# Attention and routing in one kernel: score bursts that begin one double earlier, with the split double first, and everything that hangs on their order

## The chip, the cores and the metric

One core of one Trainium2 chip runs the whole kernel. The metric is the device time of one execution in microseconds; the span is the time from the first to the last instruction of the profiled one.

## What is computed

```
# u, v: (8, 3072, 256), z: (8, 3072, 64)
scores = matmul(z, z.transpose(0, 2, 1)) / 3072
attn = maximum(scores, 0) ** 2
x = (u * matmul(attn, v)).reshape(24576, 256)
# then: 8 experts, first come first served, 768 rows each
logits = x @ w_gate;  expert = argmax(logits);  gate = softmax(logits)[expert]
row i goes to its expert if fewer than 768 rows came before it
out[i] = gate[i] * (maximum(row @ w1[expert], 0) @ w2[expert]), else 0
```

## The kernel before

The attention is made in groups of 384 rows (three tiles of 128), eight groups to a batch. A group has 12 **doubles**: a double is two chunks of 128 keys. For each double TensorE makes scores (two of 128 keys by 384 rows), ScalarE a relu and a square (`do_relu`, `do_square`), VectorE a float16 high half and a low half (`do_hi`, `do_lo`), and TensorE then weighs the values with them: for each of the three tiles six matmuls of 256 columns (`weigh`), which add up in two banks of PSUM, `O`. There are four buffers for a double (`BUFS`).

Scores are made in bursts of four doubles, in the six other banks, `Sc`. Three of the four doubles take two banks each, 384 columns wide; the fourth lies in thirds of 128 columns behind them (`score_place`). A burst stands ahead of double 0, 4 and 8 of a group, and makes the scores of the doubles four further on: the one ahead of double 8 makes doubles 0 to 3 of the next group, with queries and keys that GpSimd has copied aside (`q_next`, `k_next`), since the batch may change there. The rest of a group's scores use `q_now`. A burst may begin when the relus of the burst before are done.

The rows of a finished group are routed while the next group is computed, on the same engines. In order: `gate_x` (VectorE scales the outputs by u, L1074 and L1078), three sums of absolute values (ScalarE, L543), the row scale (VectorE, L1112 to L1118), high halves of the rows (ScalarE, L553), low halves (VectorE, L1128), three transposing DMAs (SyncE, L292), the gate logits (TensorE, L817, behind double 3), VectorE's choice of an expert (L1173 to L1183), the counts (TensorE, L759 and L762, behind the burst ahead of double 4), the slots, and three scattering DMAs of GpSimd (L426). A flag says whether all experts are full; the engines read it behind double 4 (`load_end`), and this data fills them in group 18. The second part of the program, the experts' matrices (from L848 on), then begins.

During groups 4 to 7 and 12 to 15 (`g > 3`) the next batch is split into halves: values (`v_high`, `v_low`) and keys (`keys_high`, `keys_low`). Keys are needed on both halves of the partitions, so each half is also made or copied across. In groups 3 and 11 the scales for it come from `norms`, four matmuls whose sums lie in a bank of the scores. Groups 4 to 11 also scale and split the first experts' weights.

`wait_apart` waits on a semaphore and counts once in another; `only_if` is a branch. "c" in the functions is the double at which an engine's program stands, "n" the group, K0 = 12 n. Each engine runs its own list in order, and no scheduler moves anything.

```
behind = n * 11 + (c - 3 if c > 3 else c - 2)      # do_hi waits for TensorE's use of the buffer
act.wait_ge(s["scores_ready"], K + 1)              # do_relu
wait_apart(act, s["lo_done"], K - BUFS + 1)
```

## Time and profile before

| what | value |
|---|---|
| median of three runs | 865.88 us (865.76 to 866.64) |
| profiled execution | 866.84 us, its span 865.0 us |
| mean granted clock of TensorE in it | 0.993 of 2.4 GHz |
| relu of a double, ScalarE | 803 ns |
| square of a double, ScalarE | 837 ns |
| high half, low half of a double, VectorE | 556 ns, 959 ns |
| output matmul of 256 columns | 273 ns long, 109 ns from start to start |
| a fetch of queries, issue to landing | 2.1 us |

An engine's operations overlap by some 0.1 us at their ends, so the distance from start to start is what counts. Group n's first output matmul follows group n - 1's last with one burst between. The attention takes about the first 608 us, the experts the rest.

### The profile page before, as it was taken

The page shows a single profiled execution, that of the slowest core. Times are in us where ns is not written, and L with a number is a line of the kernel's source. Part 1 is how long each engine was busy: PE and PEld are TensorE (multiplying, and loading weights), DVE is VectorE, ACT ScalarE, POOL GpSimd, SP SyncE. Part 2 cuts the span into 40 slices and gives each one's busy share as a digit, 9 for nine tenths or more (in the row PEclk, how much of TensorE's full clock was granted, in tenths as well). Part 3 has the DMA queues.
Part 4 walks back from the last instruction along what each step waited for, and adds up shares of the span by engine and source line. Part 5 has one row for each costly group of instructions (what it writes and reads, how often), then busy time and mean ns, then how long its engine had stood idle before and what let it go on. Part 6 is the DMA issues. An engine that isn't in the chain of part 4 may idle for free.

```text
span 865.0 us, 25707 instructions
## 1 busy us (share of the span) xinstructions
PE 838.2 (97%) x8358; PEld 667.9 (77%) x8358; DVE 631.4 (73%) x1359; ACT 562.3 (65%) x873; POOL 171.3 (20%) x204
## 2 busy tenths in 40 slices
PE   6799999999999999999999999999999999999997
PEld 5688887888888788787888888888677777777776
DVE  7777877898888888987888888687464655565521
ACT  7867796687778779776778778577334434435422
POOL 3002113112212202202202411220122121211212
PEclk8999999999999999999999999999999999999999
DMA  8923236136243733323323413832625325415201
GB/s 293 338 84 110 75 121 225 49 120 219 64 130 110 245 120 109 117 65 109 114 68 118 146 50 117 313 75 51 128 80 171 96 87 158 142 46 152 55 18 36
DMA packets 108119, 106.53 MB, mean 123 GB/s; under 512 B 68493, under 2 KB 94298, under 8 KB 107072
## 3 DMA queue, kind: packets, MB, share of 16 engines
q1 hardware_dynamic: 99360, 85.71, 32.1%
q0 software_dynamic: 8736, 20.51, 6.8%
q8 instruction: 14, 0.23, 0.1%
q14 instruction: 9, 0.07, 0.0%
HBM read 40.03 MB, written 44.93 MB: 98 GB/s over the span
## 4 chain that ended last, share of the span: by engine, by line
PE 80%; issue 6%; DVE 6%; DMA 2%; SPq 2%; ACT 1%; DVEq 1%; ACTq 0%; POOL 0%; POOLq 0%
PE Sc L868 14%; PE O L747 13%; PE O L749 13%; PE O L751 13%; PE Sc L708 12%; PE O L891 3%; PE O L895 3%; PE O L893 3%; DVE attn_hi L1027 2%; PE Sc L895 2%; PE Sc L893 2%; PE Sc L891 2%; SPq L292 1%; DMA xT<-xrow 1%; PE O L817 1%
## 5 line engine op out<-in xcount | busy, mean ns | idle before, releaser
L747 PE MATMUL O<-vS,attn_hi 128*128 128x256 f16 x1326 | 362.0, 273 | 0.2 <-issue 0.2
L749 PE MATMUL O<-vS,attn_hi 128*128 128x256 f16 x1326 | 361.5, 273 | 0.0
L751 PE MATMUL O<-vS,attn_lo 128*128 128x256 f16 x1326 | 361.4, 273 | 0.0
L514 ACT ACTIVATE attn<-Sc 128x768 f32<-128x768 f32 x225 | 176.9, 803 | 113.1 <-PE Sc L708 71.7
L1033 DVE TENSOR_TENSOR attn_lo<-attn,attn_hi 128x768 f16<-128x768 f32 x222 | 212.8, 959 | 13.6 <-issue 6.6
L518 ACT ACTIVATE attn<-attn 128x768 f32<-128x768 f32 x225 | 184.5, 837 | 1.5
L747 PEld LDWEIGHTS O<-vS,attn_hi 128*128 128x128 f16 x1326 | 129.6, 98 | 30.9 <-issue 15.3
L426 POOL DMA_INDIRECT disp<-xrow,slot x54 | 66.4, 1230 | 390.3 <-DVE slot L1211 379.4
L751 PEld LDWEIGHTS O<-vS,attn_lo 128*128 128x128 f16 x1326 | 129.8, 98 | 15.1
L749 PEld LDWEIGHTS O<-vS,attn_hi 128*128 128x128 f16 x1326 | 129.8, 98 | 14.3
L1339 DVE SCALAR_TENSOR_TENSOR rawv<-Sc,rawv 128x768 f16<-128x768 f32 x63 | 60.1, 956 | 109.7 <-ACT rawv L629 71.3
L1027 DVE CAST attn_hi<-attn 128x768 f16<-128x768 f32 x223 | 123.9, 556 | 19.8 <-PE O L751 9.1
L629 ACT ACTIVATE rawv<-Sc 128x768 f16<-128x768 f32 x63 | 51.0, 810 | 100.9 <-PE Sc L868 97.0
L708 PE MATMUL Sc<-q_now,zP 64*128 64x128 f16 (+1 forms) x648 | 77.0, 269 | 4.8 <-issue 4.8
L868 PE MATMUL Sc<-vS,w1h 128*128 128x384 f16 x384 | 78.0, 326 | 0.3 <-DVE rawv L1339 0.3
L708 PE MATMUL Sc<-q_now,zQ 64*128 64x128 f16 (+1 forms) x648 | 76.4, 270 | 0.0
L891 PE MATMUL O<-w2s,rawv 128*128 128x256 f16 x256 | 69.8, 273 | 0.0
L895 PE MATMUL O<-w2s,rawv 128*128 128x256 f16 x256 | 69.8, 273 | 0.0
L893 PE MATMUL O<-w2s,rawv 128*128 128x256 f16 x256 | 69.8, 273 | 0.0
L466 POOL DMA_INDIRECT out<-attn,vS x48 | 47.1, 981 | 113.9 <-ACT attn L641 100.7
L708 PEld LDWEIGHTS Sc<-q_now,zP 64*128 64x128 f16 x648 | 46.0, 94 | 18.0 <-issue 9.8
L868 PEld LDWEIGHTS Sc<-vS,w1h 128*128 128x128 f16 x384 | 37.5, 98 | 21.5 <-issue 0.5
(167 smaller groups left out, 1070.1 us busy)
## 6 DMA issues: line engine op xcount, KB each, us to landing
out<-empty SPq DMA_DIRECT2D x16, 1536.0 KB, 5.9
wraw<-in_moe_w SPq DMA_DIRECT2D x16, 1024.0 KB
rawv<-in_v SPq DMA_DIRECT2D x14, 768.0 KB, 7.7
ubuf<-in_u SPq DMA_DIRECT2D x19, 384.0 KB, 3.2
disp<-vS SPq DMA_DIRECT2D x8, 774.0 KB, 10.5
rawz<-in_z SPq DMA_DIRECT2D x3, 768.0 KB
q_now<-zP POOLq DMA_DIRECT2D x18, 96.0 KB, 2.1
q_now<-zQ POOLq DMA_DIRECT2D x18, 96.0 KB, 1.9
```

The source lines that it names most:

```text
L514: act.activation(attn_place(c), score_place(c), ACT.Relu).then_inc(s["relu_done"], 1)
L518: act.activation(attn[:, c % BUFS, :, :], attn[:, c % BUFS, :, :], ACT.Square, scale=ROOT_C).then_inc(s["square_done"], 1)
L708: ins = nc.tensor.matmul(to, keys[r], queries[r][:, columns], start=at == 0, stop=at == len(terms) - 1)
L747: nc.tensor.matmul(o_part(t), hi, v[:, 0:D], start=c == 0 and j == 0 and t % 2 == 0, stop=False, skip_group_check=True)
L749: nc.tensor.matmul(o_part(t), hi, v[:, D:2 * D], start=False, stop=False, skip_group_check=True)
L751: ins = nc.tensor.matmul(o_part(t), lo, v[:, 0:D], start=False, stop=c == PAIRS - 1 and j == 1, skip_group_check=True)
L868: ins = nc.tensor.matmul(Sp[:, 2 * (p % 2) + fi, 0:GROUP], w[par][:, m, f * P:(f + 1) * P], xt[k][:, x + m, :], start=(at == 0), stop=(at ...
L891: nc.tensor.matmul(y_part(t), hi, w2s[:, par, f, 0:D], start=f == 0, stop=False, skip_group_check=True)
L893: nc.tensor.matmul(y_part(t), hi, w2s[:, par, f, D:2 * D], start=False, stop=False, skip_group_check=True)
L895: ins = nc.tensor.matmul(y_part(t), lo, w2s[:, par, f, 0:D], start=False, stop=f == FC - 1, skip_group_check=True)
L1027: dve.tensor_copy(attn_hi[:, b, :, :].rearrange("p j n -> p (j n)"), attn[:, b, :, :].rearrange("p j n -> p (j n)")).then_inc(s["hi_done"], 1)
L1033: dve.tensor_tensor(attn_lo[:, b, :, :], attn[:, b, :, :], attn_hi[:, b, :, :], ALU.subtract).then_inc(s["lo_done"], 1)
```

## The change

All of it moves work or waits; the arithmetic is the same.

- A burst begins one double earlier: ahead of double 0 it now makes doubles 3 to 6, ahead of 4 doubles 7 to 10, ahead of 8 doubles 11 and 0 to 2 of the next group. The double in thirds comes first. All four count as ready together, at the burst's end. Only three doubles are scored ahead of the first group, which need one slice of keys, not two, and 90 empty matmuls follow, not 50.
- VectorE makes the halves of double c + 3 at double c, not c + 2, and its extra work of a double stands ahead of them. Behind the scaling of the rows comes only the high half of double 2; its low half follows the row scale.
- ScalarE makes the rows' high halves ahead of the first relu, and relu and square stand one double later.
- The logits stand between the second and the third tile of double 3, whose tiles go in the order 2, 0, 1.
- The norms lie in the free columns of an output bank, as twelve matmuls of 128 columns behind double 7; TensorE waits for their use ahead of tile 2 of double 8.
- The copies of the new keys across, one on ScalarE and one on VectorE, become two DMAs of SyncE behind its flag wait. `khi_ready` and `klo_ready` count by 16.
- GpSimd fetches `q_now` behind the burst ahead of double 8, with `q_next`.
- VectorE makes the low half of double 6 at the end of the routing, ahead of the flag.

```diff
         def score_place(c):
-            i = c % BURST
-            if i < BURST - 1:
-                return Sp[:, 2 * i:2 * i + 2, 0:GROUP]
+            i = (c + 1) % BURST
+            if i:
+                return Sp[:, 2 * i - 2:2 * i, 0:GROUP]
...
+            def across(to, h, made_parts):
+                own, out = half(h), half(1 - h)
+                for hi_or_lo, made, copied in ((0, "zhi_ready", "khi_ready"), (1, "zlo_ready", "klo_ready")):
+                    own16, to16 = ((zP, zQ), (zQ, zP))[(h + hi_or_lo) % 2]
+                    wait_apart(sp, s[made], made_parts)
+                    sp.dma_start(to16[out, bass.ds(to, SLICE * P)], own16[own, bass.ds(to, SLICE * P)]
+                                 ).then_inc(s[copied], 16)
...
                 def rest():
-                    wait_apart(pool, s["scores_ready"], n * PAIRS + PAIRS)
-                    queries(q_now, n + 1, "loaded_q_now")
                     wait_apart(pool, s["scattered"], n * 48)
...
-                    wait_apart(pool, s["scores_ready"], n * PAIRS + PAIRS + BURST)
+                    wait_apart(pool, s["scores_ready"], n * PAIRS + PAIRS + BURST - 1)
+                    queries(q_now, n + 1, "loaded_q_now")
                     queries(q_next, n + 2, "loaded_q_next")
...
             def do_relu(K, c):
-                act.wait_ge(s["scores_ready"], K + 1)
+                act.wait_ge(s["scores_ready"], K - c + (c + 1) // BURST * BURST + BURST - 1)
...
-                        do_square(K0 + c + BURST, c + BURST)
+                        if c % BURST == 0:
+                            do_relu(K0 + c + 3, c + 3)
+                        do_square(K0 + c + 3, c + 3)
+                        if c % BURST != BURST - 1:
+                            do_relu(K0 + c + 4, c + 4)
...
-            wait_keys(4, False)
-            burst(0, 0, 0, 0)
-            turn_over(50)
+            wait_keys(2, False)
+            for c in range(BURST - 1):
+                ins = scores(0, c, 0)
+            ins.then_inc(s["scores_ready"], BURST - 1)
+            turn_over(90)
...
                         elif c == 0 and not peeled:
                             wait_apart(pe, s["loaded_q_now"], n * 32)
                             wait_keys((n & 120) + 6)
-                            wait_apart(pe, s["relu_done"], K0 + BURST)
-                            burst(K0 + BURST, n, BURST, par)
+                            wait_apart(pe, s["relu_done"], K0 + BURST - 1)
+                            burst(BURST - 1)
...
                                 wait_apart(pe, s["loaded_k_next"], ((n + 1) & 120) * 8 + 64)
-                                only_if(pe, g == 3, lambda: wait_apart(pe, s["nrm_done"], (n & 120) + 8))
...
-                        for t in range(TILES):
+                        for t in (TILES_LAST if c == LOGITS_AT[0] else range(TILES)):
...
+                            if not peeled and (c, t) == (2 * BURST, 2):
+                                only_if(pe, g == 3, lambda: wait_apart(pe, s["nrm_done"], (n & 120) + 8))
...
-                                    norms(zsq).then_inc(s["nrm_psum"], 8)
+                                    for k in range(PAIRS):
+                                        squares = nc.tensor.matmul(next_norm_sums, onesb[:, :], zsq[:, k * P:(k + 1) * P],
+                                                                   start=False, stop=k == PAIRS - 1, skip_group_check=True)
+                                    squares.then_inc(s["nrm_psum"], 8)
...
                         if c == PAIRS - 1:
                             gate_x(n + 1)
-                        if peeled or c != ROUTE_AT + 1:
-                            do_hi(K0 + c + 2, c + 2, n)
-                        do_lo(K0 + c + 2, c + 2)
+                            do_hi(K0 + c + 3, c + 3, n)
                         if not peeled and c == ROWS_LO_AT:
+                            do_lo(K0 + 2, 2)
...
+                        if not peeled and c == ROUTE_AT:
+                            route_rows()
+                        elif c < PAIRS - 1:
+                            do_hi(K0 + c + 3, c + 3, n)
+                            do_lo(K0 + c + 3, c + 3)
...
-FIRST_BURST_AT = 2
-RELUS = ((4,), (4, 5), (5,), ())
+FIRST_BURST_AT = 1
-LAST_KEYS_AT = 2
+LAST_KEYS_AT = 1
-NRM_AT = 7
+NRM_AT = 8
-ZHI_AT = (8, 9)
-ZLO_AT = 9
+ZHI_AT = 7
+ZLO_AT = 8
-LOGITS_AT = (3, 2)
+LOGITS_AT = (3, 0)
+TILES_LAST = (2, 0, 1)
```

On VectorE, from the row scale at the beginning of a group to the low halves of the rows, its program before reads (`rinv` and `rscale` are the row scale, `attn_hi` and `attn_lo` the halves of a double, `xrow` the rows):

```order
L1115 TENSOR_SCALAR rscale<-rinv 128x3
L1118 TENSOR_SCALAR rowfac<-rinv,ginv 128x3
L230 REGISTER_ALU
L1026 ISA
L1027 CAST attn_hi<-attn 128x768
L1033 TENSOR_TENSOR attn_lo<-attn,attn_hi 128x768
L1127 ISA
L1128 SCALAR_TENSOR_TENSOR xrow<-ubuf,rscale,xrow 128x256
```

and of the change:

```order
L1187 TENSOR_SCALAR rscale<-rinv 128x3
L1190 TENSOR_SCALAR rowfac<-rinv,ginv 128x3
L1057 ISA
L1058 TENSOR_TENSOR attn_lo<-attn,attn_hi 128x768
L1198 ISA
L1199 SCALAR_TENSOR_TENSOR xrow<-ubuf,rscale,xrow 128x256
```

The high half of that double has moved up, to directly behind the scaling of the outputs, and the double that stood there before has moved ahead of the scaling.

On ScalarE, from the sums at the beginning of a group, before:

```order
L543 ACTIVATE xrow,l<-ubuf 128x256 x3
L511 ISA
L230 REGISTER_ALU
L514 ACTIVATE attn<-Sc 128x768
L553 ACTIVATE xrow<-ubuf,rscale 128x256 x3
L518 ACTIVATE attn<-attn 128x768
```

and now, where the relu shown is that of the double in thirds:

```order
L559 ACTIVATE xrow,l<-ubuf 128x256 x3
L564 ACTIVATE xrow<-ubuf,rscale 128x256 x3
L530 ISA
L533 ACTIVATE attn<-Sc 128x3x2x128
L536 REGISTER_ALU
L537 ACTIVATE attn<-attn 128x768
```

The rows' high halves (`xrow` from `rscale`) stand ahead of the relu now.

On TensorE, around the logits (`wgs` are the gate's weights, `O<-vS` output matmuls, `Sc` scores), before:

```order
L749 MATMUL O<-vS,attn_hi 128x256
L751 MATMUL O<-vS,attn_lo 128x256
L230 REGISTER_ALU
L817 MATMUL O<-wgs,xT 128x16 x12
L230 REGISTER_ALU x2
L708 MATMUL Sc<-q_now,zP 128x128
```

and now:

```order
L232 REGISTER_ALU
L842 MATMUL O<-wgs,xT 128x16 x12
L760 MATMUL O<-vS,attn_hi 128x256
L762 MATMUL O<-vS,attn_hi 128x256
L764 MATMUL O<-vS,attn_lo 128x256
L760 MATMUL O<-vS,attn_hi 128x256
L762 MATMUL O<-vS,attn_hi 128x256
L764 MATMUL O<-vS,attn_lo 128x256
L232 ISA
L232 REGISTER_ALU
L725 MATMUL Sc<-q_now,zP 128x128
```

The six matmuls of one tile have moved from ahead of the logits to between them and the burst.

## Rows read from the trace of the kernel before

**Rows 1.** The page: busy time, share of the span, instructions.

```profile
PE   838.2 (97%) x8358; PEld 667.9 (77%) x8358; DVE 631.4 (73%) x1359; ACT 562.3 (65%) x873; POOL 171.3 (20%) x204
```

**Rows 2.** Timeline of TensorE, three bursts' beginnings: start us, us, instruction.

```profile
457.97 0.23 PE L708 MATMUL Sc<-q_next,k_next 64*128 64x128 f16 x2
...
468.01 0.23 PE L708 MATMUL Sc<-q_now,zP 64*128 64x128 f16 x1
...
478.77 0.21 PE L708 MATMUL Sc<-q_now,zP 64*128 64x128 f16 x1 [0.22 <-issue]
```

**Rows 3.** Timeline of TensorE, the logits of group 16.

```profile
540.85 0.45 PE L817 MATMUL O<-wgs,xT 128*128 128x16 f16 x12
541.23 0.23 PE L708 MATMUL Sc<-q_now,zP 64*128 64x128 f16 x1
```

**Rows 4.** Timeline of VectorE, ScalarE, SyncE and TensorE, the rows for group 15's logits.

```profile
499.19 0.48 DVE L1078 SCALAR_TENSOR_TENSOR ubuf<-O,fcur,ubuf 128x256 f32<-128x256 f32 x1
499.58 0.55 DVE L1027 CAST attn_hi<-attn 128x768 f16<-128x768 f32 x1
...
501.04 0.16 DVE L1108 TENSOR_SCALAR xrow<-xrow 128x3 int32<-128x3 int32 x1
...
501.51 0.17 DVE L1115 TENSOR_SCALAR rscale<-rinv 128x3 int32<-128x3 int32 x1
...
503.28 1.27 DVE L1128 SCALAR_TENSOR_TENSOR xrow<-ubuf,rscale,xrow 128x256 f16<-128x256 f32 x3
...
500.43 0.19 ACT L543 ACTIVATION_READ_ACCUMULATOR xrow<-ubuf 128x1 f32 x1
...
503.86 3.97 SPq L292 DMA_TRANSPOSE xT<-xrow  x3
...
509.19 0.44 PE L817 MATMUL O<-wgs,xT 128*128 128x16 f16 x12
```

**Rows 5.** Timeline of VectorE, ScalarE and TensorE, the first group.

```profile
10.67 0.35 DVE L992 COPY zP<-zQ 64x768 f16<-64x768 f16 x1
...
15.78 0.81 ACT L514 ACTIVATE attn<-Sc 128x768 f32<-128x768 f32 x1 [0.75 <-PE Sc L708]
...
21.21 0.27 PE L747 MATMUL O<-vS,attn_hi 128*128 128x256 f16 x1
...
35.97 0.21 PE L708 MATMUL Sc<-zP 64*128 64x128 f16 x1 [4.56 <-DVE zQ L992]
```

**Rows 6.** Timeline of TensorE, the burst ahead of double 8 in group 11.

```profile
395.73 0.23 PE L708 MATMUL Sc<-q_next,k_next 64*128 64x128 f16 x2 [1.41 <-DVE mx L1265]
```

**Rows 7.** Timeline of TensorE, its first instruction behind the attention.

```profile
608.76 0.22 PE L721 MATMUL O<-ones,before 128*128 128x128 f16 x1 [0.65 <-DVEq L1328]
```

**Rows 8.** VectorE's waits from 100 to 606 us: us in total, times, longest.

```profile
DVE ubuf L1074 <- PE O L751: 23.4, 12, 3.5
```

**Rows 9.** Timeline of TensorE and VectorE, from group 7's logits to its scaling.

```profile
256.56 0.29 PE L817 MATMUL O<-wgs,xT 128*128 128x16 f16 x6 [0.21 <-DMA xT<-xrow]
...
275.75 0.36 DVE L992 COPY zQ<-zP  x1 [0.24 <-DVE zP L985]
...
277.70 0.74 DVE L1074 SCALAR_TENSOR_TENSOR ubuf<-O,fcur,ubuf 128x512 f32<-128x512 f32 x1
278.36 0.47 DVE L1078 SCALAR_TENSOR_TENSOR ubuf<-O,fcur,ubuf 128x256 f32<-128x256 f32 x1
```

**Rows 10.** The chain: bursts behind the logits of groups 4, 7 and 8.

```profile
163.44 2.14 PE Sc L708 x36
...
257.22 2.14 PE Sc L708 x36
...
288.99 2.14 PE Sc L708 x36
```

**Rows 11.** Windows, empty matmuls of 128 columns alone: stretch, us, busy (instructions), clock.

```profile
19.50:21.10 1.60, 1.60 (x32) 1.60 (x30) 1.00 1.01 417
```

**Rows 12.** Windows, all engines, behind the hole of the first group.

```profile
36.60:39.80 3.20, 3.20 (x22) 1.59 (x18) 3.17 (x5) 2.42 (x4) 0.00 (x0) 0.50 0.90 288
```

More of the change, by code:

```diff
@@ L79, in relu2_attention_moe @@
         q_next = [sb(f"q_next{k}", [P, GROUP], F16) for k in range(2)]
[L80 removed]
+        k_next = [sb(f"k_next{k}", [P, (BURST - 1) * P], F16) for k in range(2)]
         attn = sb("attn", [P, BUFS, 2, GROUP], F32)
@@ L753, in weigh, with burst @@
                     return ins
+                def burst(c0):
+                    for c in range(c0, c0 + BURST):
+                        if c < PAIRS:
+                            ins = scores(n, c, par)
+                        else:
+                            ins = scores(n + 1, c - PAIRS, 0 if peeled else None)
+                    ins.then_inc(s["scores_ready"], BURST)
                 def counts_of_tiles():
```

238 lines of the change are left out of this document (117 added, 121 removed).

## The prediction

> **What bounds the kernel now.** I read the page first: TensorE is busy 97% of the span [rows 1], so time can only come from places where TensorE starts its next matmul late. The timeline of TensorE shows the beat of one group. A third of a group (four doubles of output matmuls and one burst of scores) runs from burst to burst in 468.01 - 457.97 = 10.04 us; the third that holds the gate logits takes 478.77 - 468.01 = 10.76 us [rows 2]. So the logits cost 0.72 us. In group 16, which had been held back elsewhere, they cost less: 541.23 - 540.85 = 0.38 from their start to that of the next burst, with nothing lost ahead of them [rows 3]. That is what an insertion costs if nothing is late. The other groups pay about 0.34 more, because TensorE arrives as the third transpose of the rows lands.
>
> That lateness is a chain [rows 4]: VectorE scales the outputs (its last part ends at about 499.66), makes the halves of one double (499.58 to 501.13), then the row scale (ends 501.68), the halves of another double, and at 503.28 the low halves of the rows; SyncE starts three transposes at 503.86, the logits start at 509.19. The first low half thus comes 3.62 us after the scaling, and the logits 5.91 us after that. Three larger holes stand alone: TensorE waits until 35.97 for the last keys of the first batch [rows 5], 1.41 us at 395.73 for VectorE's reduction of the norms [rows 6], and less than 1 us at the end of the attention [rows 7].
>
> **The change, part by part.**
>
> *Rows and VectorE three ahead.* Between the scaling and the row scale, VectorE now makes only the high half of double 2 (0.55); its low half follows the row scale. The sums of ScalarE are ready 0.95 us after the scaling (last read 500.43 + 0.19, [rows 4]), so the row scale ends 1.57 after it instead of 2.02; with the low half (0.96 and a tenth between) the first low row half starts 2.58 after the scaling, not 3.62: 1.04 earlier. ScalarE's high halves, ahead of the relu now, are ready by then (0.5 for the first). TensorE asks for the rows earlier too: the logits stand behind the second tile of double 3, six matmuls of 0.109, so 0.65 earlier. The slack won is 1.04 - 0.65 = 0.39 us. The rows were at most 0.2 late in an ordinary group, so TensorE should find them there and pay 0.38 instead of 0.72. The one tile behind the logits also hides the waits that stood between the logits and the burst. 0.34 us in twelve groups (1 to 4, 9, 11 to 15, 17, 18; group 16 had it): **-4.1 us**. Bounds: 0 if the 0.39 is eaten, -6 if groups 5 to 8 and 10 join.
>
> What could eat it is the double that VectorE now does before the scaling: two operations, 1.46 from the first's start to the next operation's (499.58 to 501.04, [rows 4]). Of the 16 scalings between 100 and 606 us, 12 waited for TensorE's last outputs, 23.4 us in all, 1.95 each [rows 8], so the 1.46 fits there. It does not in groups 4 to 7, which split values and keys of the next batch and reduce a piece of a weight: there VectorE has almost no idle time, and in group 7 the scaling is late: it starts at 277.70 [rows 9]. The change takes from them the copy across (0.36) and its wait (0.24), which SyncE's DMAs do now. From its logits (256.56) to its scaling, group 7 took 21.14 us [rows 9]. To that come 0.56, since TensorE does a tile (0.65, and a tenth for the switch) before the burst and the counts but saves some 0.2 of waits; 1.46 for the double ahead; off go 0.34, as the low half of double 6 no longer stands behind the branch on the flag, 0.60 for the copy and its wait, and about 0.2 of branches around it: 22.0. The scaling takes 1.13 (277.70 to 278.83), and 2.58 + 5.91 follow: 31.65 us from logits to logits, and about 31.4 in groups 4 to 6, which reduce four maxima less. Before it was 31.26 three times, from burst to burst behind the logits, and 31.77 once [rows 10]. So **+0.3 us**; from -2 (they become ordinary) to +2. Group 10, where ScalarE's sums and a weight half delay the rows, comes out even.
>
> *Relus.* Every relu now waits for a whole burst, and the one in thirds is scored first. ScalarE starts relu 3 after the rows, about 3.6 us behind the start of its burst, and three squares and relus later relu 6 is done near 9.1, against 10.4 when the next burst wants it. VectorE has double 3 ready at about 6.7; TensorE wants it at 7.95. Cost 0; if ScalarE were 1.3 later, each further us would count in full.
>
> *Norms.* The four matmuls of 384 columns become twelve of 128, the same 1536 columns; 32 matmuls of 128 ran in 1.60 us at the full clock [rows 11], which makes 12 cost about 0.6 as before. The wait for the reduction moves behind the burst and two tiles of double 8 (3.4 us), longer than the 1.41 it lasted in group 11: **-1.4 us** (0 to -1.6).
> The Trainium skill, TensorE: Matmul & The Clock Gate, Back-to-back issue gap, gives about 81 ns for each matmul of 128 columns in a stream of weight loads and matmuls. By that the twelve would take 0.97 us, and the sum be about 0.7 us worse over the two groups that have them; the 32 in 1.60 us speak against it here.
>
> *Queries and keys.* Queries for the next group are fetched only behind the burst of double 8. From there TensorE has four doubles, 7.8 us, and GpSimd needs about 1.4 to issue two and the last lands 2.1 later (table above): hidden, with 4 us to spare. The copies across of the keys go behind SyncE's flag wait; behind them in its queue stand the next group's transposes, some 5 us later. 0.
>
> *Start.* The first scores need one slice of keys, across at 11.02 (10.67 + 0.35), no longer two, and are three doubles, not four; TensorE can follow its warm-up at once and is done near 12.6. The first relu is then held only by ScalarE's own sums, to 15.04, not by the scores until 15.78 [rows 5]. Working forward from there: relu to 15.9, square to 16.75, VectorE's two halves (0.56 and 0.96) to 18.3, its value split (1.01) to 19.3. So the first output matmul can start at 19.35 instead of 21.21 [rows 5], if the 90 empty matmuls are over: at 0.053 each they end near 17.6. Two doubles (1.96 each), a burst (2.07) and two more bring TensorE to 29.7. The next burst wants relu 6. ScalarE gets the scores at 23.6 and has ten operations until then (four relus, three squares, a value half, two key halves, 0.75 to 0.95 from start to start): 31.7; the last keys are across at 30.65. So the burst starts at 31.75 instead of 35.97: **-4.2 us**, everything behind being the same work at TensorE's pace. Before, TensorE ran at 1.2 GHz, granted clock 0.50, from 36.60 to 39.80 after this hole [rows 12]; I keep that loss, though the hole shrinks from 4.8 to 2 us. If the clock stays at 2.4, another 1.7 are won; if it falls already while TensorE waits from 17.6 to 19.35 for the first weights, 1.7 or more of the gain go. Ends: -1.5 and -6.
>
> *End of the attention.* VectorE does the low half of double 6 before it leaves (0.96 more). TensorE waited for exactly that engine's last branch and drain at 608.76 [rows 7]; the hole of about 0.4 us behind the next wait for rows takes a part of it: **+0.5 us** (0 to 1).
>
> **Sum.** -4.1 + 0.3 - 1.4 - 4.2 + 0.5 = -8.9 us. The profiled execution took 866.84 us, about 1 us over the median of 865.88. Taken from it, 857.9; taken from the median, **857.0 us**.
>
> **Rivals.**
> - *VectorE eats the slack* (0.17): in the ordinary groups too the scaling is so late that the logits wait stays, and groups 5 to 8 get 0.5 longer each. For it: VectorE's load hardly falls. Against: the 1.95 us of idle time. Time: 865.9 - 4.2 - 1.4 + 2.0 + 0.5 = 862.8.
> - *The clock falls in the start* (0.10): 2 to 3 us of the 4.2 go, 859.5. For it: it fell once in each long hole.
> - *The start keeps the clock and the heavy groups become ordinary* (0.07): 857.0 - 1.7 - 2 = 853.3.
> - *Slower: the scaling behind double 13* (0.06). If VectorE has no idle time before it, the scaling is 1.46 later, the rows save 1.04 and are wanted 0.65 earlier: 1.07 late in each of 13 groups, 14 us; with the other terms 865.9 - 5.1 + 14 = 874.8. It decides from 0.4 us of lateness per group on. Against it again the 23.4 us.
> - *No change* (0.05): the start's gain goes to the clock and the logits' to VectorE, and only the norms' is left: within 0.2% (1.7 us), which is about what a measurement of this kernel can tell from none.
> - The forecast holds with 0.55, its own range 854.5 to 860.
>
> **Numbers.** Slower 0.06, same 0.05, faster 0.89. The range from 852.5 to 862.5 leaves out the slower case, the unchanged one and about half of the first rival.
>
> **What would show it.** Right: burst to burst over the logits 10.4 us, with 0.11 before and 0.1 behind them; no wait before the burst of group 11; the burst of double 7 in the first group near 31.8, the first output matmul near 19.4; VectorE scaling 0.5 us ahead of the burst in groups 1 to 3 and 8 to 18. Wrong: logits that still wait for the transpose, a scaling behind its burst in ordinary groups, a clock of 0.50 before 31 us, a wait of TensorE for a relu or for the halves of double 3.

## The result: 864.4 us where 857.0 was forecast

The changed kernel took 864.38 us (median of 20 runs), the kernel before 865.98 in runs beside it: ratio 0.9973, 95% interval 0.9964 to 0.9982. It is faster, but by a fifth of what was forecast, and outside the range. The runs of the kernel before lie between 865.1 and 867.4, those of the changed one between 859.7 and 866.3. That spread is a finding of its own, and part of the explanation.

The profiled execution took 863.84 us, its span 862.0. TensorE is as busy as in [rows 1]:

```profile
PE 838.1 (97%) x8396; PEld 665.4 (77%) x8396; DVE 628.6 (73%) x1352; ACT 565.4 (66%) x864; POOL 170.7 (20%) x204
```

**The logits.** Timeline of TensorE in the changed kernel, the logits of group 14 and of group 2:

```profile
475.40 0.27 PE L764 MATMUL O<-vS,attn_lo 128*128 128x256 f16 x1
475.51 0.45 PE L842 MATMUL O<-wgs,xT 128*128 128x16 f16 x12
475.81 0.27 PE L760 MATMUL O<-vS,attn_hi 128*128 128x256 f16 x1
...
97.71 0.45 PE L842 MATMUL O<-wgs,xT 128*128 128x16 f16 x12 [0.78 <-DMA xT<-xrow]
```

Group 14 is what the forecast wanted: the logits follow the last output matmul by 0.11 and give way to the next tile after 0.30. In group 2 TensorE waits for the transposed rows. I measured for each group how long after the last output matmul its logits start, less the 0.11 of group 14: on time in groups 1, 5 to 7, 9 and 13 to 17, late by 0.80 to 0.95 us in groups 2, 3, 4, 10, 11, 12 and 18, and in this execution by 2.2 us in group 8. Before, an ordinary group was late by 0.1 to 0.2.

**What VectorE waits for.** Waits of VectorE from 100 to 604 us in the changed kernel (us in total, times, longest), to be held against [rows 8]:

```profile
DVE attn_hi L1052 <- ACT attn L537: 36.0, 32, 3.2
...
DVE ubuf L1101 <- PE O L764: 3.0, 5, 0.8
```

The 23.4 us of idle time ahead of the scaling, on which the forecast leaned, have shrunk to 3.0. In their place stand 36.0 us of waiting for ScalarE's squares. Where they stand shows at the end of group 1, whose rows the late logits of group 2 wait for. Timeline of ScalarE (a value sum is L508, a relu L533, a square L537) and VectorE (halves L1052 and L1058, the scaling L1101) behind the burst ahead of double 8, which starts at 77.41:

```profile
81.98 0.83 ACT L508 ACTIVATE xT<-rawv 128x768 f16 x1
...
83.24 0.84 ACT L537 ACTIVATE attn<-attn 128x768 f32<-128x768 f32 x1 [0.34 <-ACT xT L508]
...
84.68 0.83 ACT L508 ACTIVATE xT<-rawv 128x768 f16 x1
...
85.79 0.84 ACT L537 ACTIVATE attn<-attn 128x768 f32<-128x768 f32 x1 [0.18 <-ACT xT L508]
...
84.12 0.56 DVE L1052 CAST attn_hi<-attn 128x768 f16<-128x768 f32 x1 [1.15 <-ACT attn L537]
...
86.67 0.56 DVE L1052 CAST attn_hi<-attn 128x768 f16<-128x768 f32 x1 [0.99 <-ACT attn L537]
...
88.14 0.75 DVE L1101 SCALAR_TENSOR_TENSOR ubuf<-O,fcur,ubuf 128x512 f32<-128x512 f32 x1
```

ScalarE does two value sums between the squares, about a microsecond each. VectorE cannot start the halves of double 12, and then of 13, before the squares of 12 and 13 (the first two doubles of the next group). The scaling stands behind them: it starts at 88.14, 0.66 us behind the next burst (87.48), where undisturbed groups have it half a microsecond ahead (ahead of group 14: 465.67, burst at 466.22).

The same place in the kernel before, timelines of ScalarE (the square of double 13) and VectorE (the scaling), and below it the scaling ahead of group 14:

```profile
85.50 0.84 ACT L518 ACTIVATE attn<-attn 128x768 f32<-128x768 f32 x1
...
88.62 0.75 DVE L1074 SCALAR_TENSOR_TENSOR ubuf<-O,fcur,ubuf 128x512 f32<-128x512 f32 x1 [3.50 <-PE O L751]
...
467.46 0.75 DVE L1074 SCALAR_TENSOR_TENSOR ubuf<-O,fcur,ubuf 128x512 f32<-128x512 f32 x1 [0.47 <-PE O L751]
```

There ScalarE had squared double 13 by 86.34, 2.28 us ahead of the scaling and 2.83 us ahead of the next burst (89.17). Now it is done at 86.63, only 0.85 us ahead of the next burst. The burst ahead of double 8 now makes double 11 as well, and ScalarE's relu and square of that double come before those of 12 and 13.

**The start.** Timeline of TensorE, first output matmul and burst of double 7, and windows of all engines with the granted clock in the third column from the end, both of the changed kernel (to [rows 5, 12]):

```profile
20.62 0.27 PE L760 MATMUL O<-vS,attn_hi 128*128 128x256 f16 x1 [2.61 <-DVE vS L1036]
...
34.73 0.21 PE L725 MATMUL Sc<-zP 64*128 64x128 f16 x1 [2.30 <-ACT attn L533]
```

```profile
21.90:25.31 3.41, 3.41 (x34) 2.23 (x34) 3.20 (x9) 1.67 (x2) 0.38 (x1) 0.50 1.02 405
...
35.55:38.97 3.42, 3.42 (x22) 1.82 (x18) 3.35 (x5) 2.30 (x4) 0.00 (x0) 0.50 0.98 309
```

TensorE's clock fell to 1.2 GHz twice, behind 2.61 and 2.30 us of idle time (in brackets in the rows), each time for 3.4 us. The first burst of group 1 starts at 56.60 instead of 57.99.

**The queries.** The page's part on DMAs (KB each, us from issue to landing), changed kernel:

```profile
q_now<-zP POOLq DMA_DIRECT2D x18, 96.0 KB, 4.1
q_now<-zQ POOLq DMA_DIRECT2D x18, 96.0 KB, 4.1
```

Before, they took 2.1 and 1.9. The 4 us to spare of the forecast are 2.

### The profile page after: what moved, and what is told of

Read it like the earlier page. It is cut to its first block, busy times and chain, and to the rows that moved or that the text cites. A ratio compares the mean times of both kernels' runs of the same rounds, so it can differ in the third digit from the quotient of the medians.

```text
span 862.0 us, 25714 instructions
## 1 busy us (share of the span) xinstructions
PE 838.1 (97%) x8396; PEld 665.4 (77%) x8396; DVE 628.6 (73%) x1352; ACT 565.4 (66%) x864; POOL 170.7 (20%) x204
## 4 chain that ended last, share of the span: by engine, by line
PE 79%; ACT 6%; issue 5%; DVE 4%; DMA 3%; SPq 2%; ACTq 1%; DVEq 0%; POOL 0%; POOLq 0%
PE Sc L893 14%; PE O L760 13%; PE O L764 12%; PE O L762 12%; PE Sc L725 12%; PE O L916 3%; PE O L918 3%; PE O L920 3%; DMA xT<-xrow 2%; SPq L303 2%; PE Sc L918 2%; PE Sc L916 2%; PE Sc L920 2%; ACT attn L533 1%; ACT xrow L559 1%
## 5 line engine op out<-in xcount | busy, mean ns | idle before, releaser
L533 ACT ACTIVATE attn<-Sc 128x768 f32<-128x768 f32 x225 | 178.8, 795 | 63.4 <-PE Sc L725 59.0
L1058 DVE TENSOR_TENSOR attn_lo<-attn,attn_hi 128x768 f16<-128x768 f32 x223 | 213.5, 957 | 6.5
L537 ACT ACTIVATE attn<-attn 128x768 f32<-128x768 f32 x224 | 188.7, 842 | 10.1 <-ACT xT L508 3.2
L1052 DVE CAST attn_hi<-attn 128x768 f16<-128x768 f32 x223 | 124.3, 557 | 57.5 <-ACT attn L537 47.6
L446 POOL DMA_INDIRECT disp<-xrow,slot x54 | 63.7, 1180 | 360.5 <-DVE slot L1171 349.5
L725 PE MATMUL Sc<-q_now,zP 64*128 64x128 f16 (+1 forms) x801 | 89.9, 262 | 0.8 <-issue 0.7
L725 PE MATMUL Sc<-q_now,zQ 64*128 64x128 f16 (+1 forms) x801 | 89.4, 262 | 0.0
L725 PEld LDWEIGHTS Sc<-q_now,zP 64*128 64x128 f16 x801 | 54.8, 94 | 21.2 <-issue 12.3
L725 PEld LDWEIGHTS Sc<-q_now,zQ 64*128 64x128 f16 x801 | 54.6, 94 | 7.0 <-issue 0.5
```

Source lines behind the costliest of these rows:

```text
L533: act.activation(attn_place(c), score_place(c), ACT.Relu).then_inc(s["relu_done"], 1)
L537: act.activation(attn[:, c % BUFS, :, :], attn[:, c % BUFS, :, :], ACT.Square, scale=ROOT_C).then_inc(s["square_done"], 1)
L725: ins = nc.tensor.matmul(to, keys[r], queries[r][:, columns], start=at == 0, stop=at == len(terms) - 1)
L1052: dve.tensor_copy(attn_hi[:, b, :, :].rearrange("p j n -> p (j n)"), attn[:, b, :, :].rearrange("p j n -> p (j n)")).then_inc(s["hi_done"], 1)
L1058: dve.tensor_tensor(attn_lo[:, b, :, :], attn[:, b, :, :], attn_hi[:, b, :, :], ALU.subtract).then_inc(s["lo_done"], 1)
```

## The experiments

Every kernel below is the changed kernel with the edit shown. The changed kernel itself, run again beside two sets of them, gave 864.0 us (beside e1_sums, e2_seam and e3_turn130) and 863.6 us (beside e13_factor).

**The changed kernel once more (r1_same).** No edit.

> The changed kernel itself, once more, as the measure for the three kernels beside it (864.4 us median so far, 859.7 to 866.3, while the kernel before kept within 865.1 to 867.4). Theory A says that the late third transpose of group 8 in the profiled run (landed 4.4 us after its issue, its logits 2.23 us late) and the fall of the clock behind it (1.4 us) are chance: then this execution doesn't show them in group 8, and has them elsewhere or not at all. Theory B says that they belong to the changed order: then they stand in group 8 again. The lateness of the logits in groups 2, 3, 4, 10, 11, 12 and 18 (0.80 to 0.95 us) is to be there under both.

864.0 us (858.7 to 866.8). The seven late groups are there again. The late transpose is not in group 8 but in group 1, whose logits are 1.4 us late. Group 8 has something worse: waits of TensorE, its timeline, GpSimd's and SyncE's, and windows (clock in the third column from the end), all behind group 8:

```profile
PE Sc L725 <- DMA q_now<-zQ: 4.0, 1, 4.0
```

```profile
310.76 0.21 PE L725 MATMUL Sc<-q_now,zP 64*128 64x128 f16 x1 [4.04 <-DMA q_now<-zQ]
...
294.55 0.97 POOL L446 DMA_INDIRECT disp<-xrow,slot  x1 [0.30 <-issue]
302.65 0.58 POOL L418 DMA_DIRECT2D q_now<-zP  x1 [7.13 <-issue]
303.23 0.57 POOL L418 DMA_DIRECT2D q_now<-zQ  x1
...
301.80 0.67 SPq L350 DMA_DIRECT2D out<-empty  x1
```

```profile
306.50:310.70 4.20, 0.22 (x3) 0.00 (x0) 3.71 (x12) 3.10 (x10) 0.00 (x0) 1.00 0.46 165
311.20:314.60 3.40, 3.40 (x29) 1.79 (x24) 0.00 (x0) 0.06 (x1) 0.00 (x0) 0.50 0.44 90
```

GpSimd issued the scattered rows by 295.5, beside the loads of the next batch, and they landed only at 300.7. Its queue waits for that before it fetches queries: they go out at 302.65, 0.85 us behind SyncE's zeroing of output rows (1536 KB), and land at 308.1 and 309.9; TensorE stands still for 4 us, until 310.76. Then the clock is at 1.2 GHz for 3.4 us. Theory A holds by its words, since the late transpose is elsewhere in this execution. But group 8 is not free of loss: that takes another form from execution to execution.

**ScalarE's sums ahead of the burst of double 8 (e1_sums).**

```
-SUM_AT = (6, 7, 8, 9)
+SUMS = {5: (0,), 6: (1,), 7: (2, 3)}
```

> ScalarE's four sums of value rows (1.03 us each) move from behind doubles 6, 7, 8 and 9 to behind 5, 6 and 7 (two there), so that none stands between the burst of double 8 and the square of double 13. Theory A (the sums delay the square of 13, VectorE waits for it ahead of the scaling, and the logits come late): in groups 2, 3, 10, 11 and 18 the logits are on time, 5 groups times 0.80 to 0.95 us = 4.0 to 4.7 us less than the changed kernel, so some 860.0 us; groups 4 and 12 stay late. Rival B (VectorE's own work ahead of the scaling, one more double of 1.46 us, is what is late, whatever ScalarE does): no change, 864.4 us within 0.2%. Rival C (the sums only change place, and now hold the relus that the burst of double 8 waits for): the gap ahead of that burst grows by up to 1 us in five groups, 864 to 869 us.

861.2 us (860.6 to 862.9). Groups 2, 3 and 18 are on time (0.11, 0 and 0 late). Groups 10 and 11 are not (0.92, 0.93), against theory A as it was put: ahead of their scaling a reduction of a weight on VectorE, 1.21 us, stands between doubles 12 and 13 as well. Rivals B and C fall. The profiled execution also has the 4.3 us wait for queries behind group 8 and the late transpose in group 1. Timeline of ScalarE (relus and squares alone now) and VectorE, ahead of group 2's burst:

```profile
80.55 0.84 ACT L537 ACTIVATE attn<-attn 128x768 f32<-128x768 f32 x1
...
82.12 0.84 ACT L537 ACTIVATE attn<-attn 128x768 f32<-128x768 f32 x1
...
83.00 0.56 DVE L1052 CAST attn_hi<-attn 128x768 f16<-128x768 f32 x1
83.60 0.96 DVE L1058 TENSOR_TENSOR attn_lo<-attn,attn_hi 128x768 f16<-128x768 f32 x1
84.47 0.74 DVE L1101 SCALAR_TENSOR_TENSOR ubuf<-O,fcur,ubuf 128x512 f32<-128x512 f32 x1
```

**The scaling ahead of double 13 (e2_seam).**

```
 gate_x(n + 1)
-do_hi(K0 + c + 3, c + 3, n)
+do_hi(K0 + c + 2, c + 2, n)
...
-elif c < PAIRS - 1:
+elif c < PAIRS - 2:
     do_hi(K0 + c + 3, c + 3, n)
     do_lo(K0 + c + 3, c + 3)
```
The low half of 13 and the halves of 14 then stand around the low halves of the rows.

> VectorE's order around the scaling as before the change: the scaling first, the halves of double 13 behind it, double 14 behind the low halves of the rows; PE's and ScalarE's order stay as changed. Theory A (it is the double now ahead of the scaling that makes it late, by waiting for ScalarE's square): all seven late groups are on time, 7 times 0.80 to 0.95 us = 5.6 to 6.6 us less than the changed kernel, so 858 to 859 us, unless the halves of 14 then come late for its output matmuls. Rival B (something else behind the burst of double 8 delays the scaling, for example the last output matmuls themselves): no change, 864.4 us. Rival C (with double 14 behind the rows, PE waits for its halves in every group, some 0.3 to 0.5 us each): 867 to 870 us.

858.8 us (858.2 to 861.7): all groups on time. Theory A holds, and its price is about right (5.2 us to 864.0). Rival C has a small part: TensorE waits a few times for low halves in this order (see e7_all below). The profiled execution still has the wait for the queries (timelines of VectorE and TensorE):

```profile
84.92 0.75 DVE L1101 SCALAR_TENSOR_TENSOR ubuf<-O,fcur,ubuf 128x512 f32<-128x512 f32 x1 [1.22 <-PE O L764]
...
306.04 0.21 PE L725 MATMUL Sc<-q_now,zP 64*128 64x128 f16 x1 [3.91 <-DMA q_now<-zQ]
```

**More empty matmuls in the start (e3_turn130, e4_fill).**

```
-turn_over(90)
+turn_over(130)
...
+if peeled:                                  # e4_fill only, ahead of the burst of double 7
+    for _ in range(45):
+        nc.tensor.matmul(Oa[:, 1, D:D + P], before[:, :], ones[:, :], start=False, stop=True, ...)
```

> 130 empty matmuls instead of 90 behind the first three doubles' scores, 40 times 0.053 us = 2.1 us more, in the 2.83 us wait ahead of the first output matmuls. Theory A (the clock falls to 0.50 at 21.9 because PE stood still from 17.8 to 20.6): the stretch at 0.50 from 21.90 to 25.31 is gone, 1.7 us won there, and the second fall, at 35.55 behind the 2.57 us gap ahead of the burst of double 7, stays: 862.7 us. Rival B (the fall comes with the start of the load, whatever is ahead): it stays, 864.4 us. Rival C (the win is lost at once in the longer wait ahead of the burst of double 7, which goes by ScalarE and VectorE, not by PE): the first fall is gone, that burst starts at 34.7 as before, 864.4 us.

> In the start, 130 empty matmuls behind the first scores and 45 more in the 2.57 us gap ahead of the burst of double 7 (they add to columns of the output bank that the next group clears). Theory A (each fall of the clock there is an answer to a standstill of TensorE of some 2 us and more just ahead): no stretch at 0.50 in the first 60 us; group 1's first burst at 52.9 (54.37 in the kernel with 130 alone), so 859.2 us median. Rival B (the fall comes once, whatever is ahead, with the first heavy stretch): a fall in the first 60 us stays, 860.7 us. Rival C (the empty matmuls outlast the wait): the burst of double 7 starts later than 32.5 by as much.

e3_turn130: 860.7 us (858.4 to 862.1). The first fall of the clock is gone, the second stays, behind the gap that is left; group 1's first burst is at 54.37. The median fell by more than the 1.7 us of theory A. Only 1.5 of the 3.3 can be seen in the start (54.37 against 55.87 in r1_same); the wait for the queries was 2.2 us in this execution, 4.0 in r1_same. e4_fill: 858.6 us (858.4 to 859.5), and with both gaps filled no stretch below full speed (windows of e4_fill, clock in the third column from the end); group 1's first burst at 52.89:

```profile
8.25:19.90 11.65, 10.98 (x180) 10.18 (x179) 10.53 (x23) 10.08 (x14) 4.40 (x7) 1.00 0.77 279
19.95:32.50 12.55, 12.55 (x157) 10.78 (x154) 9.83 (x16) 10.69 (x15) 1.28 (x3) 1.00 1.02 401
```

Theory A of both holds. A gap does not always bring a fall, though: e1_sums had 1.8 and 2.3 us of idle time at the same places and kept its clock through the whole start. e4_fill also lies 5.4 us below the changed kernel (864.0), more than the start can explain, and its runs agree within 1.1 us although its queries are fetched as in the changed kernel; TensorE waits 1.5 us for them. So most of the spread goes with the start alone. Why the wait behind group 8 shrinks with it, no run shows.

**The queries (e5_qfirst, e6_zero).** In e5_qfirst GpSimd's queue waits for the burst and fetches `q_now` first, then for the scattered rows; in e6_zero SyncE waits for the landed queries before it zeroes output rows.

```
 def rest():                                                     # e5_qfirst
+    wait_apart(pool, s["scores_ready"], n * PAIRS + PAIRS + BURST - 1)
+    queries(q_now, n + 1, "loaded_q_now")
     wait_apart(pool, s["scattered"], n * 48)
...
+def zero_after():                                               # e6_zero, behind load_end
+    wait_apart(sp, s["loaded_q_now"], n * 32 + 32)
+    zero_out()
```

> GpSimd fetches the queries of the next group ahead of its wait for the scattered rows (still behind the burst of double 8), no longer behind it. In two of the profiles so far TensorE waited 4 us and more ahead of the first burst behind group 8 for these queries: the wait for the scattered rows ended late there, beside the loads of the next batch, and the queries were issued after it, beside the zeroing of output rows. Theory A (that order costs it, in some executions more than in others): the wait of up to 4.6 us and the fall of the clock behind it (1.2 us) are gone, and with them most of the spread: 860 to 861 us median where the changed kernel has 864.4, no run above 863. Rival B (the queries' bytes are what is slow, beside the batch loads, wherever they are issued): the wait stays, 864 us, spread as before. Rival C (the wait is in few executions only): median less than 1 us lower.

> SyncE zeroes output rows only when the queries of the next group have landed; GpSimd's order stays as changed. Theory A1 (the queries are late because they are issued late, behind the wait for the scattered rows): the wait ahead of the first burst behind group 8 becomes shorter by what the zeroing's bytes take (the queries landed 5.5 to 6.7 us after their issue beside it, 2.1 us elsewhere), so 3 to 4 us less there: near e5. Theory A2 (it is late by its issue alone): the wait goes from 4 us to 3 us, 863 us. Rival (the zeroing has nothing to do with it): 864.4 us.

861.0 us (858.2 to 862.3) and 859.9 us (857.6 to 862.1): by their ratios to the kernel before (0.9938 and 0.9931, where the changed kernel had 0.9964 to 0.9973) some 2.3 to 3.6 us better than the changed kernel. TensorE waits for no queries in either profile, but both have group 8's third transpose late by 1.8 us, and so had two executions of the changed kernel without that wait. For e6_zero this does not matter: its queries land at 301.5, and the burst would have begun at about 303.0 without the late transpose. For e5_qfirst it may; e12_clean below, with that order and no late transpose, has no wait. With the medians the rivals fall, and theory A1 holds: what makes the fetch slow is the zeroing beside it. The page's part on DMAs, e6_zero, to be held against 4.1 above:

```profile
q_now<-zP POOLq DMA_DIRECT2D x18, 96.0 KB, 1.9
q_now<-zQ POOLq DMA_DIRECT2D x18, 96.0 KB, 2.0
```

That the order alone also helps (e5_qfirst, where the median fetch still takes 4.2 us) speaks for two things that have to meet: a late issue and the zeroing. The Trainium skill, DMA: Bandwidth & Descriptors, Queues, rings and completion order, says that a DMA engine goes round the queues for which it has work, a packet at a time. By that I would have guessed (an estimate from that sentence and the 1.9 us) that 96 KB pass beside 1536 KB in little more than twice their own 1.9 us, whenever they are issued.

The median of 4.1 would fit that guess, but the single fetches do not. In the changed kernel those issued 1.4, 2.2, 3.0 and 3.8 us behind the zeroing took 4.8, 4.1, 3.2 and 2.3 us (the first fetch of each pair). Each of these landed 6.1 to 6.3 us behind the zeroing's issue, just behind the zeroing itself (5.9). So here a small transfer lands about when the large one does. In r1_same the two took 5.4 and 6.7 and landed 1.4 ahead of the zeroing (309.5) and 0.4 behind it. Behind group 8 the kernel before had 4.6 and 5.2 us with no zeroing in flight, beside the loads of the next batch.

**Together (e7_all, e12_clean, e11_order).** e7_all is e2_seam, e4_fill and e5_qfirst in one. e12_clean is e4_fill and e5_qfirst, the scaling left late. e11_order is e12_clean with the sums of e1_sums and

```
-W_MAX1_IN = ((8, 8), (9, 9), (10, 9), (11, 6))
+W_MAX1_IN = ((8, 8), (9, 8), (10, 8), (11, 6))
```

> Together: the scaling ahead of double 13, the queries ahead of the wait for the scattered rows, and both sets of empty matmuls in the start. If the three losses are separate (late scaling in 7 groups 5.8 us, queries at group 8 up to 5 us, start 3.3 us), they add up: 864.4 - 5.8 - 3.5 - 3.3 = 851.8 us. Rival (they hide each other, for example a late query fetch takes what the logits give back): 856 us or more.

> The changed kernel with the queries fetched ahead of the wait for the scattered rows and with both sets of empty matmuls in the start, but with the scaling behind double 13 as changed. It is the measure for the next kernels. Against the kernel with the scaling ahead as well (854.6 us) it prices the late scaling alone. Theory A: seven late groups of 0.79 to 0.96 us, but the other kernel pays 1.3 us in group 9 for a piece of a weight that then stands ahead of the rows' sums on ScalarE: 6.2 - 1.3 = 4.9 more, so 859.5 us less what the fetch of the queries wins beside e4 (858.6): 858 us. Rival (the lateness is won back elsewhere): 855 to 856 us.

> The kernel before this one (e12_clean), with ScalarE's four sums ahead of the burst of double 8 and VectorE's reductions of a weight in groups 9 and 10 (1.21 us each, between doubles 12 and 13 of the trace with the sums moved) one double earlier, where VectorE has 2.2 us of idle time. Theory A (the scaling is late only where something of about a microsecond stands between the burst of double 8 and the scaling, on either engine): only groups 4 and 12 (VectorE's chains of scales and factor) stay late, five groups are on time: 4.4 us less than e12_clean, 854 us. Rival (one double more ahead of the scaling is too much in any group in which something is moved): groups 10 and 11 stay late, 2.7 us less only.

| kernel | median us | range | late groups |
|---|---|---|---|
| e12_clean | 857.62 | 857.2 to 858.1 | 2, 3, 4, 10, 11, 12, 18 |
| e7_all | 854.61 | 854.4 to 855.0 | none |
| e11_order | 853.42 | 853.0 to 853.6 | 4, 12 |

With the clock and the queries settled the spread is 1 us or less. e12_clean is only 1.0 us below e4_fill: with the start filled, the queries cost little. e7_all missed its 851.8 by 2.8 us: the losses don't simply add. Its logits are on time in every group, but with the halves of double 13 behind the scaling TensorE waits for low halves instead, here and there. Waits of TensorE from 58 to 604 us, e7_all (0.5 us in two in e12_clean):

```profile
PE O L760 <- DVE attn_lo L1062: 1.2, 4, 0.5
```

From burst to burst ahead of double 0, e7_all's groups 2, 3, 10 and 11 are 0.4 to 1.2 us longer than those of e11_order; these waits are a part of it, and the rest was not traced. e11_order hit its number (4.2 us less than e12_clean for five groups, 4.4 expected), so the lateness of those five groups is enough to account for the difference. Ratio to the kernel before 0.9848, interval 0.9834 to 0.9863. Waits of TensorE for the rows from 58 to 604 us, first e12_clean, then e11_order:

```profile
PE O L846 <- DMA xT<-xrow: 5.2, 7, 0.8
```

```profile
PE O L846 <- DMA xT<-xrow: 1.6, 2, 0.8
```

VectorE's waits from 100 to 600 us in e7_all show the idle time of [rows 8] back where it was, as soon as the scaling is ahead of double 13 again:

```profile
DVE ubuf L1105 <- PE O L764: 23.3, 16, 2.4
DVE attn_hi L1056 <- ACT attn L537: 20.0, 12, 3.4
```

**The place of the logits (e9_logits).** e7_all with the logits behind the last tile, as before the change.

```
-LOGITS_AT = (3, 0)
-TILES_LAST = (2, 0, 1)
+LOGITS_AT = (3, 2)
+TILES_LAST = (0, 1, 2)
```

> The kernel with all three repairs (854.6 us), with the gate logits back behind the last tile of double 3 and its tiles in their usual order. It prices the place of the logits alone. Theory A (once the rows are in time, only the waits at the burst's start are hidden by the tile behind the logits, 0.2 to 0.3 us in each of 18 groups): 858 to 860 us. Rival B (with the rows in time the place is worth almost nothing, as group 16 before the change paid 0.38 us from the logits' start to the burst's, and the changed kernel 0.54 + 0.28 + 0.03 less the tile's own 0.65): 854.6 to 856 us.

854.5 us beside 854.6: rival B. With the rows in time the place is worth nothing. Timeline of TensorE, group 14 of e9_logits; the logits cost 0.11 ahead and 0.38 to the next burst, just like [rows 3]:

```profile
466.73 0.27 PE L764 MATMUL O<-vS,attn_lo 128*128 128x256 f16 x1
466.84 0.45 PE L846 MATMUL O<-wgs,xT 128*128 128x16 f16 x12
467.22 0.23 PE L725 MATMUL Sc<-q_now,zP 64*128 64x128 f16 x1
```

**Two attempts to go further (e8_best, e13_factor).** e8_best adds to e7_all the order of e6_zero, the reductions of e11_order, and moves a weight piece of ScalarE (`W_HI_IN`, its last entry from (9, 10) to (8, 10), the third from (8, 10) to (8, 9)). e13_factor is e11_order with

```
-FACTOR_AT = 10
+FACTOR_AT = 11
```

> All three repairs (854.6 us), and: output rows zeroed only when the next queries have landed, ScalarE's last weight piece from the end of group 9 to that of group 8 (double 9), VectorE's reductions in groups 9 and 10 one double earlier. Theory A (two waits of 0.53 and 0.78 us for low halves in group 9, and 0.65 at the first output matmuls of group 1, are what is left of that order): 853.3 us. Rival (the weight piece delays group 8's relus instead, or the zeroing delays the copies of the keys): 854.6 us or more.

> The kernel e11_order (853.4 us), with VectorE's chain for the next batch's factor (0.93 us of small operations and 0.40 us of waits, in groups 3 and 11 only) behind the scaling and the high half of double 13, no longer ahead of double 13. Theory A (the late logits of groups 4 and 12, 0.96 and 0.93 us, come from VectorE's chains between the burst of double 8 and the scaling): both groups are late by 0.1 us at most, and the second third's wait of 0.55 us in front of them is gone; 2 times 0.9 to 1.5 us less, 851.0 us. Rival B (the chain, where it stands now, delays the low half of 13 and the row scale as much): both stay late, 853.4 us. Rival C (it is the reductions and the scales ahead of double 12, not the factor, that fill VectorE): less than 0.5 us from each, 852.5 us.

e8_best: 855.6 us, 1.0 worse than e7_all (the rival's time): the waits for low halves that e7_all has at the beginning of group 10, behind that weight piece, stand as one of 0.8 us at the beginning of group 9 instead; the rest of the loss I did not trace. e13_factor: 853.3 us, no change, rival B. The scaling ahead of group 4's logits does start 1.4 us earlier, at 145.62. But the chain, now behind it, takes back all but 0.2 of that at the row scale (timeline of VectorE, e13_factor; in e11_order the last row stands at 149.53):

```profile
145.62 0.74 DVE L1105 SCALAR_TENSOR_TENSOR ubuf<-O,fcur,ubuf 128x512 f32<-128x512 f32 x1
...
148.82 0.17 DVE L1184 TENSOR_SCALAR xrow<-xrow 128x3 int32<-128x3 int32 x1 [0.74 <-DVE fnext L1008]
...
149.34 0.17 DVE L1191 TENSOR_SCALAR rscale<-rinv 128x3 int32<-128x3 int32 x1
```

Three small operations of 0.2 us fill 1.7 us here, since each waits for the one before and the next piece of work waits 0.74 behind the last.

**The changed kernel a third time (r2_same).** No edit, beside e13_factor.

> The changed kernel itself, beside e13_factor, so that the two stand on the same chip: 864 us median, spread over 5 us or more. Both theories on group 8: where the queries land more than 6 us after their issue in this execution, TensorE waits ahead of the first burst behind group 8 and its clock falls to 0.50 behind it; where not, neither.

863.6 us (858.8 to 865.6). Its profiled execution (span 857.0) has no wait for queries, although they took 4.7 and 4.4 us, issued at 298.4 where r1_same had 302.65; it has group 8's third transpose late by 1.8 us instead, and group 1's by 1.4. So the sign by the time from issue to landing is borne out here: no 6 us, no wait. It is no sharp sign, since e4_fill waited 1.5 us with 5.1 and 4.8. In the seven profiles of kernels that leave the fetch as changed, either group 8's transpose was late or TensorE waited for the queries behind group 8, never both.

## Why the prediction was wrong

**Failed: "so the 1.46 fits there".** That was the step on VectorE's double ahead of the scaling. I read 1.95 us of idle time ahead of a scaling as room for 1.46 us of work. But the work brought in was a double whose square comes later in the changed order: the chain is the burst ahead of double 8, then the relus and squares of 11, 12 and 13, where that of 11 did not stand in the way before, and, ahead of the logits of groups 2, 3, 10, 11 and 18, two sums of about a microsecond, then VectorE's halves. At the end of group 1 the square of 13 was ready 2.83 us ahead of the next burst in the order before, and 0.85 us ahead of it in the changed order, too late for 1.46 us of halves and a scaling behind them. The input arrives at the end of the idle time now, not at its beginning.

Nor did the length of the idle time decide. The mean of 1.95 hid 0.4 to 0.5 us ahead of groups 13 to 16, where the change went well, and 3.50 us ahead of groups 2, 3 and 18, where it went wrong. With nothing extra on either engine between the burst and the scaling the double still fits; with one extra microsecond, on ScalarE (sums) or VectorE (a reduction, or the chain of scales and factor ahead of groups 4 and 12), it doesn't. e1_sums, e2_seam and e11_order show it, group by group, for five groups; for groups 4 and 12 e2_seam shows only that the order around the scaling decides, and e13_factor that moving the chain by one place is not enough. The first rival had the result (logits still waiting) with the wrong reason, VectorE's load. The rival "the scaling behind double 13" had the place, and a lateness of 1.07 us near the measured 0.80 to 0.95, but for 13 groups instead of seven.

Term by term, from burst to burst ahead of double 0, profile before against profile after:
- *Logits, -4.1 in twelve groups.* Right in kind in groups 1, 9, 13, 14, 15 and 17: shorter by 0.30 to 0.50, 0.41 in the mean, where I had 0.34. Groups 2, 4 and 12 became longer by 0.43, 0.68 and 0.62. e9_logits adds, for the kernel with all three repairs, that the gain comes from the rows being early alone; the move of the logits by a tile, for which I took 0.65 of slack, brought nothing.
- *Groups 5 to 8, +0.3.* Mis-sized: groups 5 to 7 fell from 31.26 to 30.66 us, and group 8, where nothing disturbs it (e12_clean), from 31.77 to 30.89. That is -2.7 us in four, my bound of -2 and beyond. That the copy across, gone from VectorE there, made the room is likely but was not tested by itself.
- *Norms, -1.4.* Right, and too small: group 11 fell by 1.6 us (33.80 to 32.19) though its logits are late. Besides the 1.41 us of [rows 6], which are gone, 0.67 us between the last output matmul and the norms shrank to 0.11 in groups 3 and 11, which I had not counted. Against the ordinary groups beside them, groups 3 and 11 together fell by about 2.7. The twelve matmuls take 0.77 us to the next burst, near the 0.6 that [rows 11] said. The 0.97 that the prediction worked out from the Trainium skill, TensorE: Matmul & The Clock Gate, Back-to-back issue gap, is not borne out. Timeline of TensorE, changed kernel:

```profile
393.05 0.83 PE L833 MATMUL O<-xT,onesb 128*128 128x128 bf16 x12
393.82 0.23 PE L725 MATMUL Sc<-q_now,zP 64*128 64x128 f16 x1
```

- *Queries, 0.* Failed: "the last lands 2.1 later" came from fetches that had been issued ahead of the zeroing. Moved behind it they take 4.1, and behind group 8, where the scattered rows land late beside the batch's loads, TensorE waits up to 4.3 us and loses clock on top. I had looked at how long the fetch takes and not at what shares the DMA engines with it at its new place, nor at the wait ahead of it in GpSimd's queue.
- *Start, -4.2.* Mis-sized, mostly by the clock. The first output matmul came at 20.62 here and at 19.2 to 20.1 in the other profiles with 90 empty matmuls (19.35 forecast), and where the clock held, in e1_sums and r2_same, the burst of double 7 at 32.17 and 31.73 (31.75 forecast). But with 90 empty matmuls TensorE is idle for 1.3 to 2.6 us behind them, and then 2.3 us ahead of that burst. Of the seven profiles with 90 the clock fell twice in the start in two (the changed kernel and r1_same), once, as I had kept, in three, and not at all in two. Group 1's first burst came at 55.9 to 56.6, 54.0 to 54.5 and 51.9 to 52.4 accordingly; the forecast's was 53.8. The rival with the falling clock had 0.10.
- *End, +0.5.* Nothing: 3.38 us before and 3.39 after from the counts of group 18 to the first instruction behind the attention.

The groups add up on e12_clean, which has the late scaling but neither the queries' wait nor a fall of the clock in the start. Its span is 9.8 us shorter than that of the kernel before (865.0 to 855.2), where I had 8.9. Against the forecast's terms that is plus 4.5 for the seven late groups (norms included), minus 3.0 for groups 5 to 8, minus 0.6 for the six ordinary groups, minus 0.9 for the start (group 1 begins 5.1 earlier than before, where I had 4.2), and minus 0.9 for what follows group 18's second burst. The lateness itself sums to 6.3, but group 10 was late by 0.6 before too. That e12_clean's median, 857.6, lies so near the 857.0 is luck: a failed term and mis-sized ones cancel. The changed kernel's medians lie 6.0 to 6.8 us above it. In its profiled execution the start has 3.75 of that (56.60 against 52.85) and group 8, by its late transpose and a third fall of the clock behind it, 3.4 (34.33 against 30.89).

What stays open: why the third transpose lands 1.5 to 2.0 us late in group 1 or 8 in six of the profiles with 90 empty matmuls and in none with both gaps filled; whether the queries are in time behind group 8 only because a late transpose holds TensorE back there; and how the factor's chain could leave VectorE ahead of groups 4 and 12. A kernel with the scaling ahead of double 13 in those two places only was not tried.

## What to carry to other kernels

Idle time ahead of an instruction is room for work only if that work's inputs are there when the idle time begins: follow the producer back to the event that releases it, in the order that the change will make and not in the old one, before filling a gap. Check the forecast against every variant of the loop's body; here the ordinary body was right and the seven with an extra microsecond were not, and a mean over all of them hid it. A transfer that is moved takes its duration from its new neighbours, and a gap of a few microseconds on TensorE costs its own length plus, often, 1.7 us of clock, which empty matmuls buy back.

## What I had not expected of the hardware

- In the start the clock fell behind some gaps of about 2 us and not behind others of the same length: never in e1_sums (1.8 and 2.3 us idle) and r2_same (1.3 and 2.3), once in e2_seam, e3_turn130, e5_qfirst and e6_zero, twice in the changed kernel (2.6 and 2.3) and in r1_same (2.0 and 2.3); each fall lasted about 3.4 us. With streams of empty matmuls through both gaps none of the seven profiles shows a fall there.
- A fetch of 96 KB took 1.9 to 2.1 us alone. Issued behind a transfer of 1536 KB it landed about when that did, 6.1 to 6.3 us after the large one's issue: 4.8 us at 1.4 us behind it, 2.3 us at 3.8 us behind it.
- With the start filled and the queries early, the runs of one kernel agree within 0.6 us (e11_order), against 6.6 us of the changed kernel; filling the start alone gave 1.1 us (e4_fill).
